# First layer: a finished row is turned and scored a quarter later and counted one quarter later; due splits are looked up at the start of a tile

## The chip, the cores and the metric

One core of one Trainium2 chip runs the whole program in one launch. The metric is device time in microseconds (us), from three timed runs of the kernel before, beside one more execution that was taken with the hardware profiler. All times in rows are microseconds from the first instruction of that profiled execution.

## What is computed

Three stages over 14336 tokens of 192 values. A causal weighted sum over 7 neighbours, by heads of 24 columns; then two mixtures of 8 experts, each expert two matrices (192x1024, ReLU, 1024x192), each token to its best expert alone.

```
x   = conv_attention(x, weight)                 # 14336 x 192
x   = moe(x):  where x @ w_skip > 0:
        e = argmax(x @ w_gate);  g = softmax(...)[e]
        x = x + g * (relu(x @ w1[e]) @ w2[e])
out = moe2(x): e = argmax(cosine(x, emb) / tau); g = softmax(...)[e]
        out = g * (relu(x @ w1b[e]) @ w2b[e])
```

The first layer's rows (about half of all tokens) must be finished before their expert of the second layer is known: each finished row is scored against the second layer's expert vectors and written to the bucket of its best expert.

## The kernel before

The attention stage fills buckets of rows in memory, one bucket for each expert. Each layer then runs over tiles of 256 rows (`TILE`), sorted by expert: 33 tiles in the first layer, 59 in the second. While PE works on a tile of the first layer it also handles the one that was finished before it; "the row" below is that finished tile. Four tiles (`NA`) of the first layer are written out ahead of the loop, the first three of the second layer likewise.

The order is written by hand, engine by engine; semaphores join them. Nothing is scheduled by a planner. In a tile of the first layer:

- TensorE (PE), `tile` at L1123: four quarters `q` of the first product (L1061, 10 matmuls each, into PSUM banks `ph`). Behind quarter 1 it waits for `tile_out` and `placed` of the tile before, and transposes that finished tile (`y_transposed`, L1090, into `pu`). Then the next tile's input is transposed (L1049, into `pt`), the finished tile is scored (`y_scores`, L1102 to L1104, from `yT_hi`, `yT_lo`, `yT_b`, back into the head of `pu`), and four quarters of the second product follow (L1072, L1077). Behind quarter 2 of these PE waits for `marked` and counts the row (`row_counts`, L1109, L1110).
- ScalarE (ACT), `tile` at L612: high parts of the four hidden quarters (`h_high`, L590), the copy of the input (L614), the high part of the transposed row (`y_high`, L595, L596), the high part of the next input (`x_high`), and `next_high` (L598): where a split of the next expert's weights is due, L405 (first matrix) or L409 (second).
- VectorE (DVE), `tile` at L930: low parts of the hidden quarters (`h_low`, L827), of the row (`y_low`, L834, L835) and of the next input (`x_low`, L821, L822); then `mark_row` (L846 to L859) finds the best expert of each token of the row; then `next_low` (L429) looks up what is due in this tile and splits the first matrix (L420, twice) or the second (L426); then `finished` (L887 to L891) makes this tile's result from the second product, and `place_row` (L869 to L874) gives the addresses of the row before, which sets `placed`.
- GpSimd (POOL) gathers tiles (L442) and scatters placed rows (L448, two DMAs for each).

A lookup is a load of one number of `tile_info` from SBUF into a register (`value_load`, L430 on DVE, L599 on ACT), with the register work around it. The first tile of an expert has the next expert's first matrix due, the second tile its second matrix. On DVE, results of short steps that depend on each other go by a wait on the engine's own semaphore (`Chain`, L24). Two tiles make one turn of the loop `each_pair` (L339), whose register work stands between the tiles of two turns.

In the second layer DVE does gate work in each tile (L957 to L972), `next_low`, then the tile's result (L981). POOL scatters it (L522), and after that makes the norm of the next tile (L508), on which that tile's `h_low` of quarter 2 depends (L963 to L966).

Of the kernel before, what the change touches and what calls it, by code (L numbers as in the profile page):

```python
# [30 lines left out]
def conv_attention_two_moe_layers(nc, x, weight, moe_w_skip, moe_w_gate, moe_w1, moe_w2,  # L31
# [12 lines left out]
    E, _, F = moe_w1.shape  # L44
# [53 lines left out]
    with ctx:  # L98
# [84 lines left out]
        SECOND = 1 << SHIFT  # L183
# [242 lines left out]
            dve.tensor_tensor(t2[:, :, 1, :], w2raw[:, :, :], t2[:, :, 0, :].bitcast(fp32),  # L426
                              ALU.subtract).then_inc(w_ready, 1)

        def next_low(dve, l, k):  # L429
            due = dve.value_load(tile_info[l][0:1, 1, bass.ds(k, 1)], min_val=0, max_val=E + SECOND * E)  # L430
            with dve.If(due > 0):
                first = dve.snap(due & (SECOND - 1), min_val=0, max_val=E)
                second = dve.snap(due >> SHIFT, min_val=0, max_val=E)
                with dve.If(first > 0):
                    split_low1(dve, first % 2, first + l * E)
                with dve.If(second > 0):
                    split_low2(dve, second % 2, second + l * E)
# [157 lines left out]
            act.activation(yT_hi[:, :], pu[:, 0:TILE], ACT.Copy)  # L595
            act.activation(yT_b[0:DR, :], pu[0:DR, TILE:2 * TILE], ACT.Copy).then_inc(layers[0]["y_high"], 1)  # L596

        def next_high(act, l, k):  # L598
            due = act.value_load(tile_info[l][0:1, 1, bass.ds(k, 1)], min_val=0, max_val=E + SECOND * E)  # L599
            with act.If(due > 0):  # L600
                first = act.snap(due & (SECOND - 1), min_val=0, max_val=E)
                second = act.snap(due >> SHIFT, min_val=0, max_val=E)
                with act.If(first > 0):
                    act.wait_ge(w_raw, (first + (l * E + 1)) * (16 * NW))
                    split_high1(act, first % 2)
                with act.If(second > 0):
                    split_high2(act, second % 2)

        def first_layer_act(act):
            L = layers[0]  # L610

            def tile(j, par, after_a_row=True):  # L612
                h_high(act, 0, j, 0)
                act.activation(x_kept[:, par], xg[:, par], ACT.Copy).then_inc(L["kept"], 1)  # L614
                h_high(act, 0, j, 1)
                if after_a_row:
                    y_high(act, j)
                h_high(act, 0, j, 2)
                h_high(act, 0, j, 3)
                x_high(act, 0, j + 2)  # L620


            tile(0, 0, after_a_row=False)
            act.wait_ge(w_raw, 2 * (16 * NW))
            split_high(act, 1)
            for j in range(1, NA):
                tile(j, j % 2)
            act.wait_ge(L["tiles_known"], 1)
            skip, full, odd = tile_counts(act, 0)
            with each_pair(act, skip, full, L["act_turn"]) as i:  # L630
                for par in range(2):
                    tile(i * 2 + (NA + par), par)
                    next_high(act, 0, i * 2 + par)
                    act.sem_inc(L["act_turn"], 1)
            with act.If(odd > 0):
                tile(full * 2 + NA, 0)
                next_high(act, 0, full * 2)
            act.sem_inc(L["act_turn"], 1)
            return full, odd

        def second_layer_act(act, full0, odd0):
# [50 lines left out]

            def tile(i, u):
                T = loop_tile(i, u)
                h_high(act, 1, T.j, 0)
                squares(T, g_sqr)
                h_high(act, 1, T.j, 1)
                tile_middle_part(T)
                next_high(act, 1, T.j)
                tile_last_part(T)  # L700

            with each_pair(act, skip, full, L["act_turn"]) as i:
# [176 lines left out]
        def first_layer_dve(dve, place):  # L879
# [14 lines left out]
            def low_parts(j):  # L894
                h_low(dve, 0, j, 0)
                h_low(dve, 0, j, 1)
                y_low(dve, j)
                h_low(dve, 0, j, 2)
                h_low(dve, 0, j, 3)
                x_low(dve, 0, j + 2)  # L900

# [28 lines left out]
            def tile(i, par):  # L930
                j = i * 2 + (NA + par)
                chain = Chain(dve, L["chain"], (j - 1) * LINKS[0])
                low_parts(j)
                mark_row(dve, j, par, chain)
                next_low(dve, 0, i * 2 + par)
                dve.wait_ge(L[f"scattered{par}"], (i + NA // 2) * (16 * SUB))
                finished(j, par, chain)
                place_row(dve, j, par, chain)
                assert chain.count == LINKS[0]
# [12 lines left out]
        def second_layer_dve(dve, full0, odd0):  # L952
# [76 lines left out]
            def tile(i, u):  # L1029
                T = loop_tile(i, u)  # L1030
                chain = Chain(dve, L["chain"], T.j * LINKS[1])
                tile_first_part(T, chain)
                tile_middle_part(T, chain, g_nrm[:, :])
                next_low(dve, 1, T.j)
                tile_last_part(T, chain)

            with each_pair(dve, skip, full, L["dve_turn"]) as i:
# [74 lines left out]
        def first_layer_pe(pe, positions):  # L1112
# [10 lines left out]
            def tile(j, par, slot, ready, x, load, behind):  # L1123
                for q in range(FC // 2):
                    first_product(pe, 0, slot, q)
                    if q == 1:

                        pe.wait_ge(L["tile_out"], j)
                        pe.wait_ge(L["placed"], j - 1)
                        y_transposed(pe, 1 - par)  # L1130
                transposed(pe, 0, x, load)
                y_scores(pe, j)
                pe.wait_ge(w_ready, ready)
                for q in range(FC // 2):
                    second_product(pe, 0, j, slot, q)
                    behind(q)
                    if q == 2:
                        pe.wait_ge(L["marked"], j)
                        row_counts(pe)

# [601 lines left out]
```

## Time and profile before

| what | value |
|---|---|
| median of 3 runs | 1209.26 us (1207.2 to 1213.47) |
| profiled execution, whole | 1211.66 us |
| its span, first to last instruction | 1210.0 us |
| mean granted TensorE clock | 0.971 |
| PE busy | 1118.9 us, 92% of the span |
| DVE busy | 745.6 us, 62% |
| ACT busy | 556.2 us, 46% |
| POOL busy | 408.3 us, 34% |

The page gives busy time by engine; the view of waits gives idle time by the pair of waiting group and releaser; the timeline gives the start and length of single instructions, with the idle time before in brackets. "issue" is time in which an engine's instruction waited for nothing that the profile shows, which includes the engine's register work. Ends of matmuls are modelled, so starts are compared with starts below.

### The profile page before, as it was taken

How to read it: one execution, taken by the hardware profiler on the slowest of the kernel's cores; microseconds unless marked ns; L12 is line 12 of the kernel's file. 1: busy time of each engine (PE TensorE's matmuls, PEld its weight loads, DVE VectorE, ACT ScalarE, POOL GpSimd, SP SyncE). 2: the span in 40 equal slices, each digit the busy share in tenths (PEclk: the TensorE clock that was granted, in tenths of full speed). 3: DMA queues.
4: the chain of work that ended last, by engine and by line, in shares of the span. 5: the costliest groups of instructions: out<-in, count | busy, mean ns of one | idle time of the engine just before them, and what ended most of it. 6: DMA issues, size and time to landing. Idle time of an engine off the chain costs nothing.

```text
span 1210.0 us, 28287 instructions
## 1 busy us (share of the span) xinstructions
PE 1118.9 (92%) x8229; PEld 1067.4 (88%) x8230; DVE 745.6 (62%) x2136; ACT 556.2 (46%) x1499; POOL 408.3 (34%) x532
## 2 busy tenths in 40 slices
PE   4999979699998999999979999999999999999996
PEld 2877769599898998998879999999999999999996
DVE  2565668567777777777665555655556555555553
ACT  2544524144434443434335545556555555555553
POOL 1077777111212121222232333333333333333332
PEclk9999859899999999999989999999999999999998
DMA  4555255403313032133042131313113113111111
GB/s 149 157 174 171 89 168 166 117 25 98 86 38 94 27 102 83 37 88 99 22 135 58 30 102 40 98 40 87 54 34 101 40 34 101 40 39 40 41 46 33
DMA packets 62986, 96.28 MB, mean 80 GB/s; under 512 B 9235, under 2 KB 49898, under 8 KB 62816
## 3 DMA queue, kind: packets, MB, share of 16 engines
q1 hardware_dynamic: 43040, 48.85, 14.3%
q0 software_dynamic: 19904, 46.89, 12.9%
q8 instruction: 24, 0.39, 0.1%
q14 instruction: 18, 0.15, 0.0%
HBM read 61.21 MB, written 36.05 MB: 80 GB/s over the span
## 4 chain that ended last, share of the span: by engine, by line
PE 58%; issue 16%; DVE 10%; POOL 7%; ACT 3%; DMA 2%; DVEq 2%; SPq 1%; POOLq 1%; ACTq 0%
PE ph L1061 26%; PE py L1072 16%; PE py L1077 8%; POOL bucket_rows L1429 4%; PE ph L1651 1%; PE ph L1652 1%; DVE w1s L420 1%; POOL out_rows L522 1%; PE pt L1049 1%; DVE y_sum L887 1%; PE pt L1050 1%; ACT h_hi L590 1%; POOL g_nrm L508 1%; PE pu L1090 1%; DMA xg<-bucket_rows 1%
## 5 line engine op out<-in xcount | busy, mean ns | idle before, releaser
L1072 PE MATMUL py<-w2s,h_hi 128*128 128x384 f32 x1472 | 445.7, 365 | 0.0
L1061 PE MATMUL ph<-xa_hi,w1s 128*128 128x256 f32 x1472 | 390.1, 287 | 18.1 <-issue 16.2
L590 ACT ACTIVATE h_hi<-ph 128x512 fp32r<-128x512 f32 x368 | 218.0, 593 | 315.3 <-PE ph L1061 311.6
L1077 PE MATMUL py<-w2s,h_lo 128*128 128x192 f32 x1472 | 349.5, 258 | 7.4 <-DVE h_lo L827 5.4
L827 DVE SCALAR_TENSOR_TENSOR h_lo<-ph,h_hi 128x512 fp32r<-128x512 f32 x368 | 251.1, 689 | 144.8 <-ACT h_hi L590 135.0
L1061 PEld LDWEIGHTS ph<-xa_hi,w1s 128*128 128x128 f32 x1472 | 281.3, 191 | 25.0 <-issue 22.6
L1061 PE MATMUL ph<-xb,w1s 128*128 128x256 f32 x1472 | 295.4, 282 | 0.0
L1077 PEld LDWEIGHTS py<-w2s,h_lo 128*128 128x128 f32 x1472 | 280.1, 192 | 13.8 <-issue 13.8
L1072 PEld LDWEIGHTS py<-w2s,h_hi 128*128 128x128 f32 x1472 | 272.5, 190 | 0.0
L1061 PEld LDWEIGHTS ph<-xb,w1s 128*128 128x128 f32 x1472 | 228.2, 191 | 0.0
L1061 PE MATMUL ph<-xa_lo,w1s 128*128 128x256 f32 x736 | 207.8, 282 | 0.0
L522 POOL DMA_INDIRECT out_rows<-work,idx_tok x118 | 118.9, 1007 | 202.1 <-issue 199.0
L448 POOL DMA_INDIRECT bucket_rows<-yrow,idx_out x66 | 65.0, 985 | 303.4 <-DVE idx_out L874 293.0
L1429 POOL DMA_INDIRECT bucket_rows<-xrow,idx_row x112 | 113.9, 1017 | 89.7 <-DVE xrow L1603 56.1
L1061 PEld LDWEIGHTS ph<-xa_lo,w1s 128*128 128x128 f32 x736 | 141.0, 192 | 0.0
L442 POOL DMA_DIRECT2D xg<-bucket_rows x89 | 54.3, 610 | 192.6 <-issue 192.6
L665 ACT ACTIVATE y_part<-py,g_gate 128x192 f32<-128x192 f32 x118 | 49.6, 420 | 90.9 <-PE py L1072 89.1
L655 ACT ACTIVATE g_exp<-xg,g_bia,g_scl 128x8 f32<-128x8 f32 x112 | 43.1, 385 | 95.4 <-DVE g_bia L966 95.4
L981 DVE SCALAR_TENSOR_TENSOR work<-py,g_gate,y_part 128x192 f32<-128x192 f32 x118 | 48.0, 416 | 51.4 <-ACT y_part L665 51.2
L963 DVE TENSOR_SCALAR g_nrt<-g_nrm,tau 128x2 f32<-128x2 f32 x56 | 12.8, 228 | 83.3 <-POOL g_nrm L508 83.3
L1451 ACT ACTIVATE xrow<-ph 128x336 f32<-128x336 f32 x64 | 28.9, 452 | 72.4 <-PE ph L1652 67.9
L1651 PE MATMUL ph<-work,h_hi 128*128 128x336 f32 x128 | 52.7, 495 | 3.2 <-DMA h_hi<-toeplitz 3.2
(248 smaller groups left out, 1509.5 us busy)
## 6 DMA issues: line engine op xcount, KB each, us to landing
xg<-bucket_rows POOLq DMA_DIRECT2D x89, 202.0 KB, 2.8
w2raw<-in_moe_w SPq DMA_DIRECT2D x16, 768.0 KB
w1raw<-in_moe_w SPq DMA_DIRECT2D x16, 512.0 KB
w1raw<-in_moe_w SPq DMA_DIRECT2D x32, 256.0 KB
work<-in_x SPq DMA_DIRECT2D x4, 1440.0 KB, 8.6
work<-in_x SPq DMA_DIRECT2D x4, 1344.0 KB, 7.8
bucket_rows<-fill SPq DMA_DIRECT2D x24, 202.0 KB, 2.9
out_rows<-work,idx_tok POOLq DMA_INDIRECT x118, 2.4
```

Source lines behind the costliest of these rows:

```text
L442: pool.dma_start(xg[:, u, :, :].rearrange("p s r -> p (s r)"), rows[bass.ds(at, TILE), :].rearrange("(p s) r -> p (s r)", s=SUB)) \
L448: pool.indirect_dma_start(out=rows, out_offset=bass.IndirectOffsetOnAxis(ap=idx_out[:, par, s:s + 1], axis=0), in_=yrow[:, par, s, :], in_ ...
L522: pool.indirect_dma_start(out=out, out_offset=bass.IndirectOffsetOnAxis(ap=idx_tok[:, T.par, s:s + 1], axis=0), in_=y_out[T.par][:, s, :], ...
L590: act.activation(h_hi[:, 2 * q:2 * q + 2, :], ph[q][:, :].rearrange("p (c t) -> p c t", c=2), ACT.Relu).then_inc(layers[l]["h_high"], 1)
L665: act.activation(y_part[:, s, :], py[s][:, D:2 * D], ACT.Copy, scale=g_gate[:, s:s + 1]).then_inc(L["y_scaled"], 1)
L827: dve.scalar_tensor_tensor(h_lo[:, 2 * q:2 * q + 2, :].rearrange("p c t -> p (c t)"), ph[q][:, :], 0.0, h_hi[:, 2 * q:2 * q + 2, :].rearra ...
L981: ins = dve.scalar_tensor_tensor(y_out[T.par][:, s, :], py[s][:, 0:D], g_gate[:, s:s + 1], y_part[:, s, :], ALU.mult, ALU.add)
L1061: ins = pe.matmul(to, w, v[:, :], start=n == 0, stop=n == len(parts) - 1)
L1072: return pe.matmul(py[s][:, 0:2 * D], h_hi[:, f, t], w2s[:, slot, f, :, :].rearrange("p c d -> p (c d)"), start=f == 0, stop=f == FC - 1)
L1077: return pe.matmul(py[s][:, 0:D], h_lo[:, f, t], w2s[:, slot, f, 0, :], start=False, stop=False)
L1429: pool.indirect_dma_start(out=rows, out_offset=bass.IndirectOffsetOnAxis(ap=idx_row[:, r, t:t + 1], axis=0), in_=xrow[r][:, t, :], in_offs ...
L1651: pe.matmul(to, band[:, h, 0:P], xin[part][:, 1:GT + 1, c], start=True, stop=False)
```

## The change

In the first layer's loop and its tiles written out ahead, PE's transposes of the finished row go from behind quarter 1 of the first product to behind quarter 2. Its scores go from ahead of the second product to behind that product's quarter 0. The counts go from behind quarter 2 of the second product to behind quarter 3, its last. ACT and DVE follow: `y_high` and `y_low` stand behind the third hidden quarter (number 2) and no longer ahead of it. The last row of the first layer, which the second layer's code handles, stays as it was.

The lookup of what is due is a function of its own, `next_due`, and stands at the start of a tile, ahead of the tile's first work, on ACT and DVE and in both layers. The test and the split stay where they were.

```diff
+        def next_due(engine, l, k):
+            return engine.value_load(tile_info[l][0:1, 1, bass.ds(k, 1)], min_val=0, max_val=E + SECOND * E)
...
         # act, first layer
+                h_high(act, 0, j, 2)
                 if after_a_row:
                     y_high(act, j)
-                h_high(act, 0, j, 2)
                 h_high(act, 0, j, 3)
...
                 for par in range(2):
+                    due = next_due(act, 0, i * 2 + par)
                     tile(i * 2 + (NA + par), par)
-                    next_high(act, 0, i * 2 + par)
+                    next_high(act, 0, due)
...
         # dve, first layer
+                h_low(dve, 0, j, 2)
                 y_low(dve, j)
-                h_low(dve, 0, j, 2)
                 h_low(dve, 0, j, 3)
...
+                due = next_due(dve, 0, i * 2 + par)
                 low_parts(j)
                 mark_row(dve, j, par, chain)
-                next_low(dve, 0, i * 2 + par)
+                next_low(dve, 0, due)
...
         # dve, second layer (act likewise)
+                due = next_due(dve, 1, T.j)
                 tile_first_part(T, chain)
                 tile_middle_part(T, chain, g_nrm[:, :])
-                next_low(dve, 1, T.j)
+                next_low(dve, 1, due)
...
         # pe, first layer
-                    if q == 1:
+                    if q == 2:
                         pe.wait_ge(L["tile_out"], j)
                         pe.wait_ge(L["placed"], j - 1)
                         y_transposed(pe, 1 - par)
                 transposed(pe, 0, x, load)
-                y_scores(pe, j)
                 pe.wait_ge(w_ready, ready)
                 for q in range(FC // 2):
                     second_product(pe, 0, j, slot, q)
                     behind(q)
-                    if q == 2:
+                    if q == 0:
+                        y_scores(pe, j)
+                    if q == 3:
                         pe.wait_ge(L["marked"], j)
                         row_counts(pe)
```

PE in the first layer's loop, around the scores, before: the last transpose of the next input, the three matmuls of the scores (they come twice), the second product.

```order
L1050 MATMUL pt<-ident,xg 64x128
L1102 MATMUL pu<-rs_a,yT_hi 128x16
L1103 MATMUL pu<-rs_a,yT_lo 128x8
L1104 MATMUL pu<-rs_b,yT_b 128x16
...
L1072 MATMUL py<-w2s,h_hi 128x384
L1077 MATMUL py<-w2s,h_lo 128x192 x2
```

The same place of the change (line numbers are those of the changed kernel, 6 higher here).

```order
L1056 MATMUL pt<-ident,xg 64x128
L1072 ISA
L1078 MATMUL py<-w2s,h_hi 128x384
L1083 MATMUL py<-w2s,h_lo 128x192 x2
L1078 MATMUL py<-w2s,h_hi 128x384 x2
...
L1108 MATMUL pu<-rs_a,yT_hi 128x16
L1109 MATMUL pu<-rs_a,yT_lo 128x8
L1110 MATMUL pu<-rs_b,yT_b 128x16
```

A whole quarter of the second product now stands between the transposes of the input and the scores.

DVE in the first layer's loop, from the loop's register work to the second low part, before.

```order
L346 COMPARE_AND_BRANCH
L347 REGISTER_ALU x2
L347 ISA
L827 SCALAR_TENSOR_TENSOR h_lo<-ph,h_hi 128x512
L826 REGISTER_ALU
L827 SCALAR_TENSOR_TENSOR h_lo<-ph,h_hi 128x512
L834 TENSOR_TENSOR yT_lo<-pu,yT_hi 128x256
L835 TENSOR_TENSOR yT_b<-pu,yT_b 64x256
L826 REGISTER_ALU
```

The same place of the change.

```order
L346 COMPARE_AND_BRANCH
L347 REGISTER_ALU x2
L347 ISA
L430 TENSOR_LOAD tile_info
L430 ISA x2
L830 ISA
L831 SCALAR_TENSOR_TENSOR h_lo<-ph,h_hi 128x512
L830 REGISTER_ALU
...
L838 TENSOR_TENSOR yT_lo<-pu,yT_hi 128x256
L839 TENSOR_TENSOR yT_b<-pu,yT_b 64x256
```

The lookup stands ahead of the first low part, and three low parts stand ahead of the row's. Behind the marks DVE had this, before:

```order
L859 SCALAR_TENSOR_TENSOR run<-restart,hot 128x24
L430 ISA
L430 TENSOR_LOAD tile_info
L430 ISA x2
L431 COMPARE_AND_BRANCH
```

In the change the branch follows the marks directly:

```order
L863 SCALAR_TENSOR_TENSOR run<-restart,hot 128x24
L433 COMPARE_AND_BRANCH
L436 REGISTER_ALU
```

The three items of the lookup are gone from between the marks and the split.

## Rows read from the trace of the kernel before

**Rows 1.** The page, part 1: busy time of each engine over the span.

```profile
PE 1118.9 (92%) x8229; PEld 1067.4 (88%) x8230; DVE 745.6 (62%) x2136; ACT 556.2 (46%) x1499; POOL 408.3 (34%) x532
```

**Rows 2.** Waits, whole span: who waited for whom: total us, times, longest.

```profile
PE pu L1090 <- DVE idx_out L874: 19.3, 14, 1.7
...
PE py L1077 <- DVE h_lo L827: 5.4, 11, 1.8
...
PE pu L1090 <- DVE yrow L891: 0.8, 1, 0.8
```

**Rows 3.** Busy time in windows, one tile each: length, PE, PEld, DVE, ACT, POOL, clock, DMA, GB/s.

```profile
445.10:456.20 11.10, 11.07 (x89) 10.72 (x88) 8.44 (x28) 5.89 (x11) 2.54 (x3) 1.00 0.14 37
456.20:468.90 12.70, 11.31 (x88) 11.02 (x89) 9.82 (x30) 5.49 (x10) 2.54 (x3) 1.00 0.08 22
468.90:481.60 12.70, 11.38 (x90) 10.86 (x89) 9.95 (x30) 4.00 (x9) 2.55 (x3) 1.00 0.61 177
481.60:492.70 11.10, 11.10 (x89) 11.00 (x90) 7.89 (x27) 3.88 (x9) 2.54 (x3) 1.00 0.18 37
```

**Rows 4.** Timeline of PE, first layer: start, length, line, [idle before, releaser].

```profile
447.46 0.27 PE L1090 MATMUL pu<-ident,yrow 128*128 128x128 f32 x1
...
450.53 0.26 PE L1102 MATMUL pu<-rs_a,yT_hi 128*128 128x16 f32 x1
...
451.20 0.42 PE L1072 MATMUL py<-w2s,h_hi 128*128 128x384 f32 x1
...
454.72 0.18 PE L1109 MATMUL pu<-hot,not_before_b 128*128 128x16 bf16 x1
...
460.21 0.33 PE L1090 MATMUL pu<-ident,yrow 128*128 128x128 f32 x1 [1.37 <-DVE idx_out L874]
```

**Rows 5.** Timeline of DVE over the same two tiles and the next.

```profile
446.97 0.17 DVE L874 TENSOR_SCALAR idx_out<-y_at 128x2 int32<-128x2 f32 x1
447.20 0.69 DVE L827 SCALAR_TENSOR_TENSOR h_lo<-ph,h_hi 128x512 fp32r<-128x512 f32 x1
...
452.49 0.17 DVE L846 TENSOR_SCALAR y_real<-yrow 128x2 f32<-128x2 f32 x1
...
454.07 0.21 DVE L859 TENSOR_TENSOR_SCAN run<-restart,hot 128x24 bf16<-128x24 f32 x1
455.48 2.36 DVE L420 TENSOR_TENSOR w1s<-w1raw,w1s 128x1024 f32 x2 [1.20 <-issue]
457.76 0.41 DVE L887 SCALAR_TENSOR_TENSOR y_sum<-py,work 128x192 f32<-128x192 f32 x1
...
459.98 0.17 DVE L874 TENSOR_SCALAR idx_out<-y_at 128x2 int32<-128x2 f32 x1
461.03 1.29 DVE L827 SCALAR_TENSOR_TENSOR h_lo<-ph,h_hi 128x512 fp32r<-128x512 f32 x2 [0.88 <-issue]
...
468.61 1.76 DVE L426 TENSOR_TENSOR w2s<-w2raw,w2s 128x1536 f32 x1 [1.44 <-issue]
```

**Rows 6.** Chain of waits, 453 to 457 us (DVEq is DVE's sequencer): start, length, what.

```profile
454.18 0.31 DVEq L430
...
454.83 0.05 DVEq L431
```

**Rows 7.** Timelines of PE and DVE ahead of the first layer's loop.

```profile
217.43 0.18 PE L1109 MATMUL pu<-hot,not_before_b 128*128 128x16 bf16 x1 [3.52 <-DVE run L859]
...
226.94 0.33 PE L1049 MATMUL pt<-ident,xg 128*128 128x128 f32 x1 [1.33 <-DMA xg<-bucket_rows]
...
218.63 0.42 DVE L887 SCALAR_TENSOR_TENSOR y_sum<-py,work 128x192 f32<-128x192 f32 x1 [1.26 <-PE py L1072]
```

**Rows 8.** Timelines of DVE and PE in two tiles of the second layer.

```profile
825.64 0.42 DVE L822 TENSOR_TENSOR xb<-pt,xb 64x256 fp32r<-64x256 f32 x1
826.56 2.36 DVE L420 TENSOR_TENSOR w1s<-w1raw,w1s 128x1024 f32 x2 [0.50 <-issue]
...
835.00 0.33 PE L1077 MATMUL py<-w2s,h_lo 128*128 128x192 f32 x1 [0.49 <-DVE h_lo L827]
```

More of the change, by code:

```diff
@@ L427, in split_low2, with next_low @@
                               ALU.subtract).then_inc(w_ready, 1)
-        def next_low(dve, l, k):
-            due = dve.value_load(tile_info[l][0:1, 1, bass.ds(k, 1)], min_val=0, max_val=E + SECOND * E)
+        def next_due(engine, l, k):
+            return engine.value_load(tile_info[l][0:1, 1, bass.ds(k, 1)], min_val=0, max_val=E + SECOND * E)
+        def next_low(dve, l, due):
             with dve.If(due > 0):
@@ L596, in y_high, with next_high @@
             act.activation(yT_b[0:DR, :], pu[0:DR, TILE:2 * TILE], ACT.Copy).then_inc(layers[0]["y_high"], 1)
-        def next_high(act, l, k):
-            due = act.value_load(tile_info[l][0:1, 1, bass.ds(k, 1)], min_val=0, max_val=E + SECOND * E)
+        def next_high(act, l, due):
             with act.If(due > 0):
@@ L631, in first_layer_act @@
                 for par in range(2):
+                    due = next_due(act, 0, i * 2 + par)
                     tile(i * 2 + (NA + par), par)
-                    next_high(act, 0, i * 2 + par)
+                    next_high(act, 0, due)
                     act.sem_inc(L["act_turn"], 1)
             with act.If(odd > 0):
+                due = next_due(act, 0, full * 2)
                 tile(full * 2 + NA, 0)
-                next_high(act, 0, full * 2)
+                next_high(act, 0, due)
             act.sem_inc(L["act_turn"], 1)
@@ L694, in tile @@
                 T = loop_tile(i, u)
+                due = next_due(act, 1, T.j)
                 h_high(act, 1, T.j, 0)
@@ L698, in tile @@
                 tile_middle_part(T)
-                next_high(act, 1, T.j)
+                next_high(act, 1, due)
                 tile_last_part(T)
```

## The prediction

> **What bounds the kernel now.** The page comes first: PE is busy for 92% of the span and no other engine for over 62% [rows 1], so time can only come out of PE's idle stretches or its clock. The waits of PE come next. The largest pair in the loops is the row's transpose (L1090) waiting for DVE's `placed`: 14 waits, 19.3 us [rows 2]. Where they sit is read from windows of one tile each. An expert has mostly four tiles here; I call them A (its first, in which DVE splits the next expert's first matrix), B (the second matrix), C and D. A and D take 11.1 us, B and C 12.7 [rows 3]. So a group of four loses 2 x 1.6 = 3.2 us, and the 14 waits are seven such groups: 22 us, somewhat more than the waits themselves, since the engine also restarts.
>
> The timeline says why. In A the transpose starts 447.46 - 445.1 = 2.35 us into the tile, which is two quarters of 1.17 [rows 3, 4], unblocked. DVE has by then long set `placed` (446.97 + 0.17) [rows 5]. But at the end of A, DVE ends its marks, idles 1.20 us, splits for 2.36, and starts the tile's result at 457.76, 1.54 into B; the addresses start 2.22 later (459.98) and PE transposes at 460.21, 1.37 late by the row [rows 4, 5]. B's split (L426, behind 1.44 idle) does the same to C. DVE is the late engine around a split, and every 1 us that PE needs the row later, or DVE reaches the split earlier, is worth up to 1 us there.
>
> **The change, part by part.** No operation is added or removed. Prices are distances between starts.
>
> *Lookup.* In A it lies between the marks and the split: the load starts at 454.18 and the branch at 454.83, 0.65 apart; the marks' last step starts at 454.07, so with the register step ahead of the load it is 0.76 at most [rows 5, 6]. I take 0.74. The rest of the 1.20 idle (branches, addresses) stays. Moved to the head of a tile, it stands behind `placed` and ahead of `h_low` of quarter 0. Does DVE's register work run beside the engine there? The row of the loop's turn says no: 0.88 idle between L874 and the next L827 where a turn lies between, while without a turn L827 starts 447.20 - 446.97 = 0.23 after L874 [rows 5]. I take the lookup at its full 0.74 there, and 0 as the other end. So DVE's own time in a tile does not shrink in the first layer; the lookup is only moved from ahead of the split to behind `placed`.
>
> The Trainium skill (Perfetto Trace Analysis, DVE / Act Engine Instruction) says that the sequencer pushes an instruction into a wait queue and is then ready for the next one. By that the moved lookup would lie under the short steps of `place_row` and cost nothing. The 0.88 us of idle time in rows 5 speak against it at this place; it is the second rival below.
>
> *Order on PE.* The transposes are wanted at 3 x 1.17 = 3.51 into a tile, not 2.35. Scores are wanted where quarter 0 of the second product ends: 450.53 - 445.1 = 5.42 before, and 5.42 - 0.03 + 1.17 = 6.56 after [rows 3, 4] (a quarter is (454.72 - 451.20) / 3 = 1.17; scores 451.20 - 450.53 = 0.67; each set of transposes 0.35). Between transposes and scores PE still does the same amount of work. But the row's low part now stands behind a third `h_low`.
>
> Walk through one group, times from each tile's start.
>
> A, nothing late before it: `h_low` of quarter 2 can start at 3.51 + 0.92 = 4.43 (0.92 is what L827 of quarter 0 shows against its quarter: 447.20 - 445.1 - 1.17), the row's low part 0.61 later and 0.85 long (the two L827 in one row of 1.29 are 0.60 apart [rows 5]; 0.85 is two steps of 0.42 like the input's low part in [rows 8]), so it is done at 5.9 against 6.56: no wait, 0.6 spare. In D a turn and the lookup come first: 1.86 + 1.05 + 0.74 = 3.65, three low parts and the row's give 6.35, spare 0.2. The marks start when scores have ended, 6.56 + 0.67 and 0.27 for the last matmul's own length [rows 4] = 7.50, against 452.49 - 445.1 = 7.39 before. So 0.1 is lost and 0.74 gained ahead of the split: the result in B starts 1.54 - 0.62 = 0.92 into B, L874 at 3.14, `placed` at 3.3. PE wants it at 3.51: the wait of 1.37 is gone.
>
> B: now DVE is what is late next. L874 at 3.14, then turn and lookup 1.05 + 0.74: `h_low` 0 at 4.93, ends 5.62; PE wants it at 3.51 + 0.36 + 1.17 + 0.35 = 5.39, a wait of 0.3. Low parts 1 and 2 and the row's: 4.93 + 3 x 0.61 + 0.85 = 7.61 against PE's 6.87, a wait of 0.8. B becomes 11.1 + 1.1 = 12.2, gain 0.5. Marks from 9.1, L426 at 9.1 + 1.58 + 1.65 - 0.74 = 11.6 (1.65 is 1.44 idle plus the marks' last 0.21), the result 1.7 later at 1.1 into C.
>
> C: L874 at 3.3, `placed` at 3.5, just in time. No turn: `h_low` 0 at 3.3 + 0.23 + 0.74 = 4.3, the row's low part done at 7.0 against 6.56: a wait of 0.4 to 0.5. C becomes 11.6, gain 1.1. D stays.
>
> A group gains 0.5 + 1.1 = 1.6, seven give 11.2 us. Where the turn stands at the other tile the two waits change places. Ends: 7 x 0.7 = 5 if DVE gives back all but the lookup's share, 7 x 2.9 = 20 if the lookup costs nothing at its new place.
>
> *Counts.* They need the marks, 1.6 + 0.2 after those start: 9.3 in A, wanted at 10.75: no wait. Behind the last quarter a late mark no longer holds the second product. That decides once, ahead of the loop: PE waits 3.52 for the marks, with quarter 3 behind it, and DVE, done with the marks, idles 1.26 for exactly that quarter (218.63) before the result. The `placed` that follows releases POOL's scatter and, behind it in POOL's queue, the gather for which PE waits again, 1.33 at 226.94 [rows 7]. In the change quarter 3 is done by then: 1.2 us earlier along this chain. Upstream the first row's wait of 0.8 [rows 2] and about as much again of shifted order go too. I take 2.3, ends 0 (the gather's landing bound by other transfers) and 3.5.
>
> *Lookup in the second layer.* The split starts 826.56, 0.50 after the input's low part ended (825.64 + 0.42), for the lookup's sake; in the change it can start at once [rows 8]. Its new place is behind the two result steps, which wait on ACT, while DVE's register work goes on; and `h_low` 0 is wanted late there. An earlier split lets the result, POOL's scatter, the norm and `h_low` 2 move up, for which PE waits 0.49 in the next tile (835.00) [rows 8]. All such waits sum to 5.4 in 11 [rows 2]. Not all are behind a split, but each that goes also spares PE's restart. I take 4, ends 0 and 7.
>
> On ACT, which is busy for 3.9 to 5.9 us of a tile [rows 3], the lookup moves into its wait for quarter 0. Nothing.
>
> Sum: 11.2 + 2.3 + 4 = 17.5 off the profiled execution's 1211.66 gives 1194.2. The median of the three runs, 1209.26, lies 2.4 lower and would give 1191.8. I take **1193 us**.
>
> **Rivals.** *The lookup is hidden at its new place.* Then the waits in B and C are 0.5 or less in all: a group gains 2.9, 20 + 2.3 + 4 = 26, **1184 us**. Against it the 0.88 of rows 5.
>
> *DVE gives it back.* B and C are bound by DVE's own work, and PE's wait only moves from the transposes to the low parts and the scores. With 0.7 a group, nothing ahead of the loop (the gather bound by other transfers) and 2 in the second layer: 5 + 0 + 2 = 7, **1203 us**. For it: DVE works without a pause from A's split to B's scores. Against: PE asks for the row 1.17 later, and D and A have room.
>
> *Slower: scores wait in every tile.* The row's low part stands behind `h_low` 2 with 0.2 to 0.6 spare. If that part of the chain (ACT's high part of the row, now behind its third quarter, and DVE behind it) is over 1.0 later than in my walk, PE waits 0.6 in each of 29 loop tiles on average, 17 us, all that is won; at 1.2 it is +6 net, **1215 us**. The price is paid 29 times, the gain 14.
>
> **How the numbers follow.** Forecast (gain 12 to 22) 0.62; lookup hidden 0.12; given back 0.15; slower 0.06; nothing measurable in sum, by a mix of the ends above, 0.05. Faster than 0.5% means below 1203.2, which is also about what a measurement can tell from no change. The forecast and the hidden lookup count as faster, with two thirds of the third case: 0.84; same 0.10; slower 0.06. The range reaches from the hidden lookup, 1184, to the third case, 1203.
>
> **What would show it.** Right: the pair L1090 behind L874 falls from 19.3 us to under 3; new waits of PE appear at the scores behind the row's low part (about 14, 0.4 to 0.8 each) and before quarter 0 of the second product; B takes 12.2, C 11.6, A and D 11.1; idle time before L420 falls from 1.20 to 0.5, and that before the first L827 of a turn grows from 0.88 to 1.6; the 3.52 ahead of the loop falls to about 2.3 and the 1.33 grows. Wrong: A or D longer than 11.2 (the slower case), the transposes still waiting (marks later than I think), or the idle time before L827 still 0.88 (the hidden lookup).

## The result

| | median us | runs |
|---|---|---|
| kernel before | 1208.23 | 1206.33 to 1213.47, 4 runs |
| changed kernel | 1194.33 | 1191.08 to 1195.24, 4 runs |
| ratio | 0.9873 | 95% interval 0.9836 to 0.991 |

Faster by 13.9 us, 1.3 us above the 1193 forecast. The gain itself is known to 2 us or so: a second series below gives 15.6 (1192.17 against 1207.76). The profiled span fell by 20.5, from 1210.0 to 1189.5. To see where, I cut both traces at the first matmul of each tile (us):

| stretch | before | changed | difference |
|---|---|---|---|
| up to the first layer's first tile | 180.24 | 175.81 | -4.4 |
| its tile 0 | 11.80 | 12.41 | +0.6 |
| tiles 1 to 4 (4 is the loop's first) | 61.94 | 59.61 | -2.3 |
| tiles 5 to 32, the rest of the loop | 333.66 | 325.23 | -8.4 |
| tiles 33 to 36, passage to the second layer | 57.32 | 55.76 | -1.6 |
| the rest of the second layer, to its last matmul | 553.41 | 549.05 | -4.4 |

Behind the last matmul both spans have 11.6 more. The first row lies in a stage that the change leaves alone. Two more profiled executions of the changed kernel start tile 0 at 176.98 and 177.55. Two kernels below that share this stage with both start it at 179.92 (order alone) and 175.33 (the kernel before, with counts moved ahead of the loop only). So this is variation between executions, and so is most of what the span shows beyond the medians. The loops repeat well: 325.23, 325.25 and 325.08 in the first layer, 549.05, 549.03 and 548.99 in the second.

### The profile page after: what moved, and what is told of

It reads as the page before. It is cut to its first block, busy times and chain, and to the rows that moved or that the text cites. A ratio compares the mean times of both kernels' runs of the same rounds, so it can differ in the third digit from the quotient of the medians.

```text
span 1189.5 us, 28287 instructions
## 1 busy us (share of the span) xinstructions
PE 1114.0 (94%) x8229; PEld 1063.4 (89%) x8230; DVE 744.8 (63%) x2136; ACT 554.2 (47%) x1499; POOL 408.4 (34%) x532
## 4 chain that ended last, share of the span: by engine, by line
PE 67%; issue 10%; DVE 10%; POOL 6%; DMA 2%; ACT 2%; DVEq 1%; SPq 1%; POOLq 0%; ACTq 0%
PE ph L1067 30%; PE py L1078 19%; PE py L1083 10%; POOL bucket_rows L1436 4%; DVE h_lo L831 1%; PE pt L1055 1%; PE pt L1056 1%; PE ph L1658 1%; DVE w1s L420 1%; PE ph L1659 1%; DVE y_sum L891 1%; DMA bucket_rows<-xrow,idx_row 1%; DMA xg<-bucket_rows 1%; POOL out_rows L524 1%; PE pu L1110 1%
## 5 line engine op out<-in xcount | busy, mean ns | idle before, releaser
L1067 PE MATMUL ph<-xa_hi,w1s 128*128 128x256 f32 x1472 | 390.9, 287 | 19.5 <-issue 17.7
L1083 PE MATMUL py<-w2s,h_lo 128*128 128x192 f32 x1472 | 348.7, 257 | 4.3 <-DVE h_lo L831 2.4
L831 DVE SCALAR_TENSOR_TENSOR h_lo<-ph,h_hi 128x512 fp32r<-128x512 f32 x368 | 248.9, 688 | 134.0 <-ACT h_hi L592 131.3
L1067 PEld LDWEIGHTS ph<-xa_hi,w1s 128*128 128x128 f32 x1472 | 280.7, 191 | 24.4 <-issue 22.0
L1067 PE MATMUL ph<-xb,w1s 128*128 128x256 f32 x1472 | 295.2, 282 | 0.0
L1083 PEld LDWEIGHTS py<-w2s,h_lo 128*128 128x128 f32 x1472 | 279.6, 192 | 9.9 <-issue 9.5
L1067 PEld LDWEIGHTS ph<-xb,w1s 128*128 128x128 f32 x1472 | 227.8, 190 | 0.0
L1067 PE MATMUL ph<-xa_lo,w1s 128*128 128x256 f32 x736 | 207.6, 282 | 0.0
L1067 PEld LDWEIGHTS ph<-xa_lo,w1s 128*128 128x128 f32 x736 | 140.6, 191 | 0.0
L968 DVE TENSOR_SCALAR g_nrt<-g_nrm,tau 128x2 f32<-128x2 f32 x56 | 12.8, 228 | 73.5 <-POOL g_nrm L510 73.5
```

The lines of the kernel that those rows point to most:

```text
L831: dve.scalar_tensor_tensor(h_lo[:, 2 * q:2 * q + 2, :].rearrange("p c t -> p (c t)"), ph[q][:, :], 0.0, h_hi[:, 2 * q:2 * q + 2, :].rearra ...
L1067: ins = pe.matmul(to, w, v[:, :], start=n == 0, stop=n == len(parts) - 1)
L1083: return pe.matmul(py[s][:, 0:D], h_lo[:, f, t], w2s[:, slot, f, 0, :], start=False, stop=False)
```

## The profile after

Busy time on the page, answering to [rows 1] (same columns): the amounts are nearly the same over a shorter span.

```profile
PE 1114.0 (94%) x8229; PEld 1063.4 (89%) x8230; DVE 744.8 (63%) x2136; ACT 554.2 (47%) x1499; POOL 408.4 (34%) x532
```

Waits of the changed kernel (who <- for whom: total us, times, longest), answering to [rows 2]. L1096 is now the row's transpose, L1108 its scores, L1067 the first product, L1083 the low half of the second.

```profile
PE ph L1067 <- issue: 17.7, 18, 5.9
...
PE pu L1108 <- DVE yT_b L839: 4.0, 7, 0.6
...
PE py L1083 <- DVE h_lo L831: 2.4, 4, 1.6
...
PEld pu L1096 <- DVE idx_out L878: 1.4, 7, 0.3
```

The 19.3 us of the transposes are gone from the matmuls; what is left of that pair is seven waits of 0.2 each on the weight load (PEld). Seven waits at the scores came in its place. The first row, idle time without a releaser, grew from 13 to 18 times and by 1.5 us.

One group in windows, answering to [rows 3]: A, B, C, D.

```profile
434.10:445.20 11.10, 11.10 (x91) 10.94 (x91) 8.80 (x28) 5.78 (x11) 2.56 (x3) 1.00 0.13 37
445.20:457.30 12.10, 11.48 (x90) 10.92 (x89) 9.28 (x29) 5.28 (x10) 2.54 (x3) 1.00 0.08 23
457.30:469.50 12.20, 11.61 (x92) 11.01 (x91) 9.96 (x31) 4.00 (x9) 2.56 (x3) 1.00 0.63 184
469.50:480.50 11.00, 11.00 (x89) 10.90 (x89) 7.55 (x27) 3.89 (x9) 2.55 (x3) 1.00 0.14 38
```

DVE over B, answering to [rows 5] (start, length, line, [idle before, releaser]):

```profile
443.95 2.36 DVE L420 TENSOR_TENSOR w1s<-w1raw,w1s 128x1024 f32 x2 [0.47 <-issue]
...
448.46 0.17 DVE L878 TENSOR_SCALAR idx_out<-y_at 128x2 int32<-128x2 f32 x1
450.26 1.89 DVE L831 SCALAR_TENSOR_TENSOR h_lo<-ph,h_hi 128x512 fp32r<-128x512 f32 x3 [1.63 <-ACT h_hi L592]
...
452.49 0.42 DVE L839 TENSOR_TENSOR yT_b<-pu,yT_b 64x256 fp32r<-64x256 f32 x1
...
456.93 1.76 DVE L426 TENSOR_TENSOR w2s<-w2raw,w2s 128x1536 f32 x1 [0.72 <-issue]
458.61 0.41 DVE L891 SCALAR_TENSOR_TENSOR y_sum<-py,work 128x192 f32<-128x192 f32 x1
```

The idle time before the splits fell (1.20 to 0.47, 1.44 to 0.72) and that before the first low part grew (0.88 to 1.63): the lookup has moved and still costs its time. The 1.63 has ACT as its releaser by name, but the chain of waits shows DVE's own sequencer there, the loop's turn (L344 to L347) and then the lookup:

```profile
448.46 0.03 DVE idx_out L878
...
449.37 0.09 DVEq L347
...
449.49 0.30 DVEq L430
...
449.82 0.20 DVEq L430
...
450.26 0.07 DVE h_lo L831
```

On PE the rows show idle time in two places: in B at the scores, and at the end of C ahead of D's first matmul.

```profile
453.05 0.25 PE L1108 MATMUL pu<-rs_a,yT_hi 128*128 128x16 f32 x1 [0.57 <-DVE yT_b L839]
...
468.82 0.17 PE L1116 MATMUL pu<-run,ones_b 128*128 128x16 bf16 x1
469.48 0.38 PE L1067 MATMUL ph<-xa_hi,w1s 128*128 128x256 f32 x1 [0.49 <-issue]
```

Ahead of the loop, answering to [rows 7]: the wait for the marks is down from 3.52, that for the gather up from 1.33.

```profile
212.60 0.18 PE L1115 MATMUL pu<-hot,not_before_b 128*128 128x16 bf16 x1 [2.37 <-DVE run L863]
...
220.90 0.33 PE L1055 MATMUL pt<-ident,xg 128*128 128x128 f32 x1 [2.93 <-DMA xg<-bucket_rows]
```

In the second layer, answering to [rows 8], the split of w1 starts as the input's low part ends, and the 0.49 of the next tile's L1083 does not come back:

```profile
807.84 0.42 DVE L826 TENSOR_TENSOR xb<-pt,xb 64x256 fp32r<-64x256 f32 x1
808.32 2.36 DVE L420 TENSOR_TENSOR w1s<-w1raw,w1s 128x1024 f32 x2
```

## The experiments

### The two halves of the change

*Order alone*: PE, ACT and DVE have the new order, the lookups stay at their old places. Against the changed kernel (ACT and the second layer likewise):

```diff
-                due = next_due(dve, 0, i * 2 + par)
                 low_parts(j)
                 mark_row(dve, j, par, chain)
-                next_low(dve, 0, due)
+                next_low(dve, 0, next_due(dve, 0, i * 2 + par))
```

> The changed kernel with the lookups back between the marks and the splits, on ACT and DVE and in both layers; only the order differs from the kernel before. My walk: the result in B starts about 1.6 into B, so the transposes still wait there and in C (0.7 to 0.9 each) and the scores in the one that has the turn (0.5); a group of four tiles gains 1.2 to 1.5 us of 47.5, seven groups 8 to 11, nothing in the second layer's loop, 1.5 to 2.5 ahead of the loop: 10 to 13 faster than the kernel before, 2 to 6 slower than the changed kernel. Rival, the lookup is what matters: then this gains under 4 in the first layer's loop.

*Lookup alone*: the lookups at the head of each tile, the order of before. Against the changed kernel (ACT likewise; PE's three places back too):

```diff
-                h_low(dve, 0, j, 2)
                 y_low(dve, j)
+                h_low(dve, 0, j, 2)
                 h_low(dve, 0, j, 3)
```

> The kernel before with the lookups at the head of a tile; the order on PE as before. Walk: the split starts 0.74 earlier, but the low parts 0.74 later; waits at the transposes fall by 0.7 in B and C, and new ones at the scores appear (0.6 in the tile with the turn): a group gains 0.7, seven 5, the second layer's loop 4, ahead of the loop 0: 8 to 9 faster than before in sum. Rival, the lookup is hidden at its new place: a group gains 1.5, 14 to 15 in sum. Rival, DVE gives all back: 4, all of it in the second layer.

Measured, with the lengths of the tiles (means of three groups):

| kernel | median us | ratio to before (95%) | first loop | second layer | A, B, C, D |
|---|---|---|---|---|---|
| before | 1206.82 | 1 | 333.66 | 553.41 | 11.11, 12.71, 12.61, 11.08 |
| order alone | 1197.6 | 0.9915 (0.9898 to 0.9932) | 323.99 | 552.91 | 11.04, 12.12, 12.03, 10.98 |
| lookup alone | 1195.67 | 0.9902 (0.9883 to 0.992) | 328.31 | 549.20 | 11.10, 12.54, 11.92, 11.18 |
| both | 1194.33 | 0.9873 (0.9836 to 0.991) | 325.23 | 549.05 | 11.09, 12.15, 12.07, 11.02 |

(The row of both is from the runs at the head.) Each half did in the loops what was expected of it: 9.7 for 8 to 11 with the order alone, 5.4 for 5 and 4.2 for 4 in the two layers with the lookup alone. As a whole the first is a little under its range (9.2 for 10 to 13), the second above it (11.2 for 8 to 9).

In the first layer the halves don't add: 9.7 and 5.4 alone, 8.4 together. With the order in place the lookup at a tile's head costs 1.2 there; all that it brings is some 4 in the second layer. PE's waits of the order alone say why it was not free at its old place either: the transposes still wait, at less than half the length.

```profile
PE pu L1091 <- DVE idx_out L875: 7.8, 14, 0.7
```

### Does the lookup cost time where it now stands?

*Lookup behind the input's low part*, in the first layer on DVE; all else as in the changed kernel.

```diff
-                due = next_due(dve, 0, i * 2 + par)
                 low_parts(j)
+                due = next_due(dve, 0, i * 2 + par)
                 mark_row(dve, j, par, chain)
```

> The changed kernel with DVE's lookup of the first layer moved from the head of the tile to behind the two steps of the next input's low part. Theory: at the head it costs 0.74 us since DVE's register work waits there for the address step to start; behind two plain steps of 0.43 each it runs beside them. Then low parts and scores of B and C come 0.7 earlier, the waits at the scores (0.57 and 0.12) and before quarter 0 go, and the loop of the first layer gains 0.7 to 1.3 for each group, 5 to 9 us against the changed kernel. Rival, register work never runs beside DVE's steps: the marks start 0.74 later, the split and the next transposes too, and nothing is gained.

Measured: 1184.51 us (1182.02 to 1188.08), ratio 0.9812 (0.979 to 0.9834), the fastest so far. The loop takes 314.36 us, 10.9 less than in the changed kernel, more than the 5 to 9 that I expected. What I had left out is C: its marks end 9.75 into the tile and no longer 10.46, and what stands behind them on TensorE moves with them (see the end of C, below). Windows of one group:

```profile
429.50:440.60 11.10, 11.10 (x91) 10.95 (x90) 8.89 (x28) 5.78 (x11) 2.56 (x3) 1.00 0.15 37
440.60:452.00 11.40, 11.32 (x91) 10.99 (x89) 9.33 (x29) 5.28 (x10) 2.54 (x3) 1.00 0.09 24
452.00:463.40 11.40, 11.30 (x91) 10.92 (x89) 9.62 (x30) 4.00 (x9) 2.55 (x3) 1.00 0.69 197
463.40:474.40 11.00, 10.99 (x87) 10.90 (x88) 7.93 (x27) 3.89 (x9) 2.54 (x3) 1.00 0.13 38
```

In B, the view of line L430 (operation, times, ns, first and last start) puts DVE's lookup at 447.2 to 447.9, and the timeline shows what the engine did meanwhile:

```profile
L430 DVEq TENSOR_LOAD <-tile_info x1: 304/304/304, 447.4 to 447.4; - x1
...
L430 DVEq SEQ_ASSERT  x1: 33/33/33, 447.9 to 447.9; - x1
```

```profile
444.92 1.89 DVE L831 SCALAR_TENSOR_TENSOR h_lo<-ph,h_hi 128x512 fp32r<-128x512 f32 x3 [0.88 <-issue]
...
447.15 0.42 DVE L839 TENSOR_TENSOR yT_b<-pu,yT_b 64x256 fp32r<-64x256 f32 x1
447.60 0.69 DVE L831 SCALAR_TENSOR_TENSOR h_lo<-ph,h_hi 128x512 fp32r<-128x512 f32 x1
448.20 0.41 DVE L825 TENSOR_TENSOR xa_lo<-pt,xa_hi 128x256 fp32r<-128x256 f32 x1
448.63 0.42 DVE L826 TENSOR_TENSOR xb<-pt,xb 64x256 fp32r<-64x256 f32 x1
449.08 0.17 DVE L850 TENSOR_SCALAR y_real<-yrow 128x2 f32<-128x2 f32 x1
```

The lookup runs while L839 and L831 do; the low parts and the marks follow each other as closely as without one (448.63 to 449.08 here, 453.97 to 454.42 in the changed kernel). The sequencer (the part of the engine that reads instructions and hands them on) was some steps ahead. Behind the row's addresses it is not: each of these steps waits for the one before. In the changed kernel the sequencer's next item stands at 448.47, where the last of them starts at 448.46; turn and lookup follow, and nothing is queued that would cover them. Two runs test this.

*Two lookups at the head*: the changed kernel, with the line `due = next_due(dve, 0, i * 2 + par)` twice.

> The changed kernel, with VectorE's lookup done twice in a row at the head of each tile of the first layer's loop. Theory (the lookup at the head holds VectorE up by its whole 0.74 us, as behind the row's addresses nothing is queued that covers it): another 0.6 to 0.74 us in the tiles B and C, where VectorE is the late engine: the scores wait 1.1 to 1.3 in B instead of 0.57 and 0.8 in C instead of 0.12; A and D have 0.2 to 0.6 spare and lose 0.1 to 0.5. A group of four loses 1.3 to 2.2 us, the loop 9 to 15, the kernel stands at 1203 to 1210. Rival (the lookup runs beside the engine at the head, and what the kernel with the lookup behind the input's low part won came from somewhere else): the second one runs beside it too, 0 to 2 us, 1194 to 1197.

*A second lookup where two plain steps stand ahead of it*, in the kernel with the lookup behind the input's low part.

```diff
                 h_low(dve, 0, j, 2)
                 y_low(dve, j)
+                due = next_due(dve, 0, i * 2 + par)
                 h_low(dve, 0, j, 3)
                 x_low(dve, 0, j + 2)
                 due = next_due(dve, 0, i * 2 + par)
```

> The kernel with VectorE's lookup behind the input's low part, and a second lookup between the row's low part and the fourth h_low, where two plain steps of 0.42 us each stand ahead of it as well. The second lookup is on the path of VectorE's low parts in B and C. Theory (a lookup costs time only where nothing is queued ahead of it on the engine: behind two plain steps of 0.85 us in all, its 0.74 is covered): 0 to 2 us, 1184 to 1187, and no idle time of VectorE ahead of the fourth h_low. Rival (the lookup always costs its 0.6 to 0.74, and behind the input's low part that only fell into a stretch in which nobody waits for VectorE): the marks end 0.7 later in B and C and the split and the result with them, 0.7 us in C and in the tile behind it, 7 x 0.7 to 7 x 1.4: 5 to 10 us, 1190 to 1195.

Beside them the changed kernel was run again:

> The changed kernel once more, on the chip and in the rounds of the next three. It gives the base for them and its own profile: 1192 to 1196 us. If the 20.5 us between the two profiled spans were all the change's, a second profiled execution would also start its first tile of the first layer near 175.8 us; I think the 4 us of them that lie ahead of that tile are variation between executions, in stages that the change doesn't touch (the kernel with the order alone started it at 179.9, before at 180.2).

| kernel | median us | ratio to before (95%) | first loop | A, B, C, D |
|---|---|---|---|---|
| changed, again | 1192.17 | 0.9877 (0.9857 to 0.9897) | 325.25 | 11.07, 12.14, 12.06, 10.99 |
| two lookups at the head | 1203.68 | 0.9963 (0.9949 to 0.9977) | 335.05 | 11.06, 12.8, 12.6, 11.07 |
| second lookup covered | 1184.59 | 0.9807 (0.9776 to 0.9838) | 313.80 | 11.04, 11.41, 11.31, 10.96 |

(B and C of the second row are from the two of the three groups at full clock, see the last section.) A second lookup at the head costs about 10 us; a second one behind the row's low part costs nothing. At the head, PE's new wait of 0.66 to 0.76 in B stands ahead of quarter 0 of the second product and not, as I had expected, at the scores, which still wait 0.57. DVE's idle time with two lookups at the head:

```profile
454.43 0.17 DVE L878 TENSOR_SCALAR idx_out<-y_at 128x2 int32<-128x2 f32 x1
456.86 1.89 DVE L831 SCALAR_TENSOR_TENSOR h_lo<-ph,h_hi 128x512 fp32r<-128x512 f32 x3 [2.25 <-issue]
```

and of the covered pair, whose first stands at 445.3 and second at 446.8, no idle time before any step:

```profile
L430 DVEq TENSOR_LOAD <-tile_info x2: 309/312/315, 445.3 to 446.8; - x2
```

```profile
446.71 0.42 DVE L839 TENSOR_TENSOR yT_b<-pu,yT_b 64x256 fp32r<-64x256 f32 x1
447.15 0.69 DVE L831 SCALAR_TENSOR_TENSOR h_lo<-ph,h_hi 128x512 fp32r<-128x512 f32 x1
447.76 0.41 DVE L825 TENSOR_TENSOR xa_lo<-pt,xa_hi 128x256 fp32r<-128x256 f32 x1
```

The idle time at the head is 0.88 with no lookup, 1.63 with one and 2.25 with two: each adds 0.62 to 0.75. So on DVE the cost of a lookup is a matter of what is queued ahead of it, which these runs show and do not only argue.

The Trainium skill (Perfetto Trace Analysis, DVE / Act Engine Instruction) has the sequencer ready for the next instruction once it has pushed one. Behind plain steps the trace agrees: the lookup of 0.6 us took no time from the engine. Behind the chained steps of `place_row` it does not, and the measurement decides: 1.63 idle.

### The end of C: TensorE's own register work

The turn was no term of the forecast. The waits for the marks and the turn's register work are both done by TensorE's sequencer (PEldq in the rows). In the changed kernel the marks of C end at 467.77; TensorE's branch L1195, the first item behind the counts, starts at 467.8, the last branch of the turn at 469.4, and D's first matmul at 469.48.

```profile
467.56 0.21 DVE L863 TENSOR_TENSOR_SCAN run<-restart,hot 128x24 bf16<-128x24 f32 x1
```

```profile
L1195 PEldq COMPARE_BRANCH  x2: 68/118/169, 467.8 to 469.4; - x2
```

So with the counts last, 1.6 us of register work start when the wait for the marks is met, covered by the matmuls that are still queued. In A the same work ended as the last matmul did, with no idle time to speak of ahead of B; C's marks come later in the tile (10.46 for 9.41). From that first branch to the next tile's first matmul it is 1.65 in this C and 1.67 in the A of the same group, which suggests that the turn sets the start of the next tile in both. Three runs asked about this.

*Counts behind quarter 2 in the loop* (behind quarter 3 ahead of it), in the changed kernel:

```diff
-                    if q == 3:
+                    if q == counts_at:
                         pe.wait_ge(L["marked"], j)
                         row_counts(pe)
```

> The changed kernel with the counts behind quarter 2 again in the loop's tiles, and behind quarter 3 only in the tiles ahead of it. Theory: PE idles 0.25 to 0.49 before the first product of the tile behind C, because its register work of the loop's turn (1.5 us) stands behind the wait for the marks (10.3 into C) and the products queued ahead of it last only until 11.8. Then that idle time goes in all groups and the loop gains 1.5 to 3 us; counts in B and C then wait about 0.1. Rival, the gap has another cause (weights, the input's low part): it stays and the time is the same or 1 us more.

*Three more register loads in the turn*, results unused:

> The changed kernel, with three more loads of a register on TensorE in the first tile of each turn of the loop, results unused. Two such loads stand 0.52 us apart in the trace of the changed kernel, so this is 1.5 us more for TensorE's sequencer at the place of the turn. Theory (the sequencer gets to the turn's register work only when the wait for the marks, behind the last quarter, has been met, and only the matmuls still queued cover it): where the idle time before the first product of D was 0.49 it becomes 1.9 to 2.0, and before B, where the register work ended just as the last matmul did, 1.2 to 1.5; the late VectorE gets up to 0.6 of that back in B. 7 x 1.5 + 7 x 0.7 to 7 x 1.5 is 15 to 21 us, 1209 to 1216. Rival (the register work runs well ahead of the matmuls, and the 0.49 has another cause, VectorE or ScalarE): 0 to 3 us, and the idle time before D stays at 0.5.

*TensorE's two loads for the next tile moved into the turn*:

```diff
                 j = i * 2 + (NA + par)
+                if par == 0:
+                    look_ahead(i * 2)
                 ready = pe.snap(ready_of, min_val=1, max_val=2 * E)
```

> The changed kernel, with TensorE's two register loads for the first tile of a turn (which weights, and whether they are ready) at the head of that tile, behind the turn's register work, and no longer under the second product of the tile before. The loads stand 0.52 us apart in the trace of the changed kernel, so the two put 1.0 us more at the place of the turn and nothing is added elsewhere. Theory (TensorE's sequencer gets to the turn only once the wait for the marks, behind the last quarter, is met, and then only the matmuls still queued cover it): the idle time before the first product of D grows from 0.45 to 1.5, and that before B from 0 to 0.9 or 1.0, of which B's wait for the scores gives back up to 0.57. Fourteen turns, 7 x 1.0 + 7 x 0.4 to 7 x 1.0: 10 to 14 us, 1202 to 1207. Rival (the turn's work is covered by the matmuls queued behind it, and the 0.45 has another cause): 0 to 3 us, and the idle time before D stays at 0.45.

The first gave 1197.28 us, ratio 0.9916 (0.99 to 0.9933): nothing won, and rather slower than the changed kernel. Its loop takes 326.46, 1.2 more. The idle time before D falls only from 0.49 to 0.29:

```profile
470.18 0.38 PE L1067 MATMUL ph<-xa_hi,w1s 128*128 128x256 f32 x1 [0.29 <-issue]
```

C is 0.16 shorter than in the changed kernel, but A is 0.13 and B 0.14 longer. Quarter 3 is now to be issued behind the same wait, ahead of the turn: in A the turn's first branch stands 9.57 into the tile and no longer 9.46. The counts themselves come a quarter earlier than the marks of B and C allow (they start 0.05 behind the marks' end there). My expectation was wrong in sign. Even so D starts 1.65 behind that branch, as before the edit. The second run had none of the three loads in its trace, as it seems because nothing used their results. It is the changed kernel once more (1191.91 us, ratio 0.9875, loop 325.08) and says nothing on the turn.

The third gave 1202.83 us, ratio 0.9956 (0.9934 to 0.9978), against 0.9877 of the changed kernel: 9.5 us more, just under the expected 10 to 14. The lines shown only add the loads; those under the second product of the tile before, whose results are now overwritten, are no longer in the trace, so their number is the same (29 of each) and the two have moved. Idle time stands where the theory puts it, before D and before B:

```profile
451.96 0.38 PE L1067 MATMUL ph<-xa_hi,w1s 128*128 128x256 f32 x1 [0.83 <-issue]
```

```profile
476.30 0.38 PE L1067 MATMUL ph<-xa_hi,w1s 128*128 128x256 f32 x1 [1.39 <-issue]
```

From the first branch behind the counts to the next tile's first matmul it is now 2.55 in C and 2.52 in A of the group shown, 0.9 more in both. A takes 11.94 and C 13.00, B only 11.27, since DVE has caught up by the time B's scores are wanted. The loop takes 7.3 us more in this trace, 1.5 of them in one D tile of 12.54 at a lower granted clock (last section), so the loads account for 5.8. The rest of the 9.5 is not in the loop and stays open. The turn does stand on TensorE's path behind the marks.

*Both edits that were tried alone*, lookup behind the input's low part and counts behind quarter 2 in the loop:

> The kernel with VectorE's lookup behind the input's low part, and besides the counts behind quarter 2 of the second product in the loop (behind quarter 3 ahead of it), that is, the two edits that were each tried alone. With the lookup there the marks end 0.2 us or more earlier in C, so that the idle time before D is 0.1 to 0.3 on average and 0.8 once: little is left for the earlier counts to win. Theory: 0 to 2 us in the loop, 1182.5 to 1184.5 where the lookup alone gave 1184.5. Rival (the counts behind quarter 2 wait for marks that come at 10.1 to 10.3 us into C, and hold quarter 3 up): 0.1 to 0.2 us in each tile behind a split, 1185 to 1187.

1186.41 us, ratio 0.9816 (0.9784 to 0.9847), loop 316.29 against 314.36: no gain over the lookup's place alone, within what can be measured, and the loop's length speaks for the rival.

### Ahead of the loop

*Counts behind quarter 3 only ahead of the loop*, in the kernel before; one run.

```diff
-                    if q == 2:
+                    if q == counts_at:
                         pe.wait_ge(L["marked"], j)
```

> The kernel before, with the counts behind the last quarter of the second product only in the three tiles ahead of the loop. Theory of the prediction (quarter 3 no longer stands behind the late marks): the wait of 3.52 for the marks falls by 1.2 to about 2.3, and the wait for the gather that follows moves 1.2 earlier, so the stretch ahead of the loop is 1.2 us shorter (61.9 to 60.7), and the loop and the second layer stay within 1 us of before. Rival (the gather's landing is set by something else): the gather's wait takes the 1.2 back, and the stretch stays at 61.9.

1205.19 us. The tile with the late marks falls from 15.39 to 13.62, the wait for them from 3.52 to 2.37, about the 1.2 expected. The two tiles behind it take 36.25 for 34.58, with 2.53 at the gather, and the stretch stays at 61.73.

```profile
213.01 0.18 PE L1109 MATMUL pu<-hot,not_before_b 128*128 128x16 bf16 x1 [2.37 <-DVE run L859]
...
222.56 0.33 PE L1049 MATMUL pt<-ident,xg 128*128 128x128 f32 x1 [2.53 <-DMA xg<-bucket_rows]
```

This one run favours the rival, the gather that takes back. But those two tiles took 35.1, 37.5 and 32.5 us in three executions of the changed kernel, so what reaches the end of the stretch stays open. That tiles 1 and 2 are 2 to 3 us shorter is firm: 24.49, 24.49 and 24.44 in three executions of the changed kernel, against 27.35 before and 26.67 in the lookup alone, which has the order of before. With the counts alone moved they take 25.49.

## Why the prediction was right, and where it was off

- **What bounds the kernel**: right. The transposes' wait went from 19.3 us to nothing on PE's matmuls, and waits at the scores came, though the view lists 7 of them and not about 14: those of C are too short for it and show only in the starts.
- **The lookup costs its 0.74 at the head**: right, and shown by both experiments on it. It was the step on which the sum hung most: with "hidden at its new place" the loop was to gain 20, and the kernel in which it really is hidden gains 19.3. (That its time, 1184.5, is the rival's 1184 is in part luck: its whole gain was 22.3 and the rival's 26.)
- **B**: 12.15 against 12.2. `h_low` of quarter 0 starts 5.06 into B (walk 4.93), the row's low part ends at 7.71 (7.61), the split starts at 11.73 (11.6). Against A, quarter 0 of the second product starts 0.34 later and the scores 1.07 later in all (mean starts 5.94 for 5.60, 7.90 for 6.83), where the walk had 0.3 and 0.3 + 0.8. The rows list only 0.57 of it as a wait, since the matmuls' ends are modelled.
- **C**: 12.07, not 11.6. This term was mis-sized: a group gains 1.1, not 1.6 (0.56 in B, 0.54 in C), the loop 8.4, not 11.2. The distances from the tile's start, means of three groups against those in A, split it. The transposes start 0.14 late (3.76 for 3.62; the result began 1.31 into C and not 1.1, so `placed` was not "just in time"). The scores start 0.46 late (7.29 for 6.83), as the walk had it with 0.4 to 0.5. The counts start 0.53 late (11.48 for 10.95), and D's first matmul 0.98. So the walk holds as far as the scores, and nearly all that it lacked, 0.45, lies behind the counts: it is the turn. The step that failed is "Counts: no wait": I priced the wait that DVE causes, and overlooked what is queued behind it on TensorE. Before, quarter 3 stood between the counts and the turn.

```profile
440.90 0.17 PE L1108 MATMUL pu<-rs_a,yT_hi 128*128 128x16 f32 x1
...
464.59 0.25 PE L1108 MATMUL pu<-rs_a,yT_hi 128*128 128x16 f32 x1
```

(The scores of A and of C in one group; the tiles start at 434.08 and 457.30.)

- **A and D**: 11.1 and 11.0 as told, so no sign of the slower case.
- **Ahead of the loop**: 2.33 against 2.3, but by luck. Tiles 1 and 2 gave 2.9, and the two behind them vary by 5 us between executions.
- **Second layer**: 4.4 against 4, and nearly all of it the lookup's: 4.2 with the lookup alone, 0.5 with the order alone.
- **The passage between the layers**: 1.6 that I didn't forecast. It repeats in the changed kernel (55.76, 55.58 and 55.62 us in three executions), but the kernel with the counts last ahead of the loop only has 55.68 there too, and the others have 57 to 61. Whether it is the change's stays open.
- **The sum**: 17.5 forecast off a profiled execution of 1211.66; the terms measured 2.3 + 8.4 + 4.4 = 15.1, the medians 13.9. The terms were 2.4 too high, by the 2.8 of the loop, nearly all of it in C. The other 1.2 are within what a median of four runs can tell; the second series gave 15.6. That the sum's 1194.2 lies so close to the measured 1194.33 is in part luck: it was taken off an execution 3.4 us slower than the median of before.

## What to carry to other kernels

On VectorE here, a scalar load into a register cost nothing behind queued steps that don't wait for each other, and its full 0.6 to 0.75 us behind a chain of steps that do: choose its place by the instructions ahead of it, not by how early it is. Moving a wait to the end of a loop body puts the loop's own register work behind it; look at what the sequencer does next, not only at the matmuls. Two edits that relieve the same late engine don't add; measure each alone and both.

## What the hardware showed that I had not expected

With two lookups at the head, the granted clock fell in two of seven B tiles, which took 14.35 and 15.90 us and not 12.8. In the windows of the second (clock third from the end) it reads 0.63 and 0.52, close to the lower level of 1.2 GHz. Up to there TensorE had run at the full clock and idled in this tile for 0.66 us ahead of the second product's quarter 0 and for 0.57 at the scores, which start at 459.65.

```profile
451.20:459.00 7.80, 7.14 (x58) 6.73 (x56) 5.37 (x14) 5.12 (x10) 2.54 (x3) 1.00 0.03 8
459.00:463.00 4.00, 3.42 (x16) 3.38 (x16) 3.52 (x15) 0.17 (x1) 0.00 (x0) 0.63 0.15 52
463.00:467.00 4.00, 4.00 (x17) 3.92 (x15) 2.43 (x3) 0.00 (x0) 0.00 (x0) 0.52 0.12 25
```

Other B tiles with idle times as long (0.74 and 0.58) kept the full clock, so the idle time alone doesn't settle it, and the cause stays open. The same came once with TensorE's loads in the turn: behind 2.09 us idle ahead of a D tile, its first 4.1 us read 0.58, and it took 12.54 us for 11.0. The groups shown of the other kernels have the full clock throughout. In B it cost 1.6 and 3.1 us. In the C behind the second, 1.5 came back (11.09 for 12.6), since DVE is no longer late.
